# The opening of a recurrent attention stage on Trainium2, written in another order

## What is computed

```python
# r, k, v: (4, 8, 768, 48); w, u: (8, 48)
for t in range(S):
    kt, vt, rt = (k[:, :, t], v[:, :, t], r[:, :, t])
    cur = np.einsum('bhd,bhe->bhde', u[None] * kt, vt)
    y[:, :, t] = np.einsum('bhd,bhde->bhe', rt, state + cur)
    state = w[None, :, :, None] * state + np.einsum('bhd,bhe->bhde', kt, vt)
# y as x: (3072, 384), a row for each token
h = x @ w_in                                   # (3072, 2048)
g = np.where(h >= 1, h, np.where(h <= -1, 0.0, (h + 1) ** 2 / 4))
x = g @ w_out                                  # (3072, 384)
# then a second layer of 8 experts with 1024 columns, one for each token
```

## Time and profile before

| | us |
|---|---|
| median of 3 runs | 768.75 (768.74 to 770.08) |
| the profiled execution | 767.32 |
| its span, first to last instruction | 765.2 |
| TensorE busy | 722.6 (94%) |
| VectorE busy | 407.1 (53%) |
| ScalarE busy | 311.4 (41%) |
| GpSimd busy | 118.6 (16%) |

### The profile page before, as it was taken

How to read it: one execution, slowest core, us unless ns; L and a number is a source line. 1 busy time by engine, 2 the same in 40 slices (tenths; PEclk the granted TensorE clock), 3 DMA queues, 4 the chain that set the end, 5 groups by cost and what they waited for, 6 DMA issues and landing times. The chain is left out here.

```text
span 765.2 us, 12834 instructions
## 1 busy us (share of the span) xinstructions
PE 722.6 (94%) x4947; PEld 607.1 (79%) x4948; DVE 407.1 (53%) x687; ACT 311.4 (41%) x545; POOL 118.6 (16%) x149
## 2 busy tenths in 40 slices
PE   5899999999999999999999999997199999999995
PEld 4688888888888888888888888885089999998995
DVE  6878786755566556655566554543644222223321
ACT  3577665434454445444454446444232212112120
POOL 6300012222221122222222100000520000000000
PEclk9999999999999999999999999999589999999998
DMA  8883122011121111011010001001520120202011
GB/s 151 210 221 74 29 53 64 12 30 33 32 73 32 33 32 56 19 32 32 11 43 2 1 1 42 1 0 43 194 97 21 63 83 1 83 1 82 20 62 41
DMA packets 88317, 40.36 MB, mean 53 GB/s; under 512 B 77113, under 2 KB 84929, under 8 KB 88257
## 3 DMA queue, kind: packets, MB, share of 16 engines
q1 hardware_dynamic: 86400, 34.61, 17.9%
q10 hardware_dynamic: 1856, 4.93, 1.7%
HBM read 30.10 MB, written 9.44 MB: 52 GB/s over the span
## 5 line engine op out<-in xcount | busy, mean ns | idle before, releaser
L946 PE MATMUL x_ps<-g_p,wout_hi 128*128 128x512 f32 x576 | 182.5, 398 | 0.2 <-DVE g_p L726 0.2
L964 PE MATMUL h_ps<-x0T,win_hi 128*128 128x512 f32 x576 | 178.3, 391 | 1.9 <-DVE x0T L654 1.9
L509 ACT ACTIVATE above<-h_ps,minus_one 128x512 f32<-128x512 f32 x96 | 66.0, 688 | 170.0 <-DVE mid L739 169.5
L964 PEld LDWEIGHTS h_ps<-x0T,win_hi 128*128 128x128 f32 x576 | 107.5, 188 | 24.7 <-DVE x0T L654 2.2
L946 PEld LDWEIGHTS x_ps<-g_p,wout_hi 128*128 128x128 f32 x576 | 104.6, 188 | 22.2 <-issue 1.4
L1503 PE MATMUL ch_ps<-x_p,w_p 128*128 128x512 f32 x432 | 109.1, 400 | 12.1 <-DVE w_p L1569 12.1
L739 DVE TENSOR_SCALAR mid<-h_ps 128x512 f32<-128x512 f32 x96 | 66.2, 690 | 98.6 <-PE h_ps L964 98.1
L946 PE MATMUL x_ps<-g_p,wout_lo 128*128 128x512 f32 x288 | 112.6, 391 | 0.0
L964 PE MATMUL h_ps<-x0T,win_lo 128*128 128x512 f32 x288 | 112.1, 389 | 0.0
L748 DVE TENSOR_TENSOR mid<-mid,above 128x512 f32<-128x512 f32 x96 | 70.8, 738 | 70.8 <-ACT mid L510 70.7
L1492 PE MATMUL cy_ps<-w_p,h_p 128*128 128x384 f32 x576 | 107.7, 336 | 0.0
(11 more groups left out here) (214 smaller groups left out, 621.4 us busy)
## 6 DMA issues: line engine op xcount, KB each, us to landing
xr<-xT_scratch SPq DMA_DIRECT2D x8, 768.0 KB, 5.0
rkv<-in_v SPq DMA_DIRECT2D x24, 192.0 KB, 2.9
xT_scratch<-xbuf ACTq DMA_DIRECT2D x6, 768.0 KB, 3.4
out<-acc SPq DMA_DIRECT2D x12, 384.0 KB, 2.4
rkv<-in_r SPq DMA_DIRECT2D x20, 192.0 KB, 3.5
rkv<-in_k SPq DMA_DIRECT2D x20, 192.0 KB, 3.7
win_raw<-in_moe_w_in SPq DMA_DIRECT2D x48, 64.0 KB, 3.3
wout_raw<-in_moe_w_out SPq DMA_DIRECT2D x4, 768.0 KB, 6.8
```

The costliest lines, as they stand in the source:

```text
L509: raises(act.activation(above[:, f % 2], h_ps[f % 2][:, :], ACT.Relu, bias=minus_one[:, :]), "over")
L946: last = pe.matmul(x_ps[kk][:, :], (wout_hi, wout_lo)[a][:, f, cols], g_p[:, at % NG, b], start=(f == 0 and n == 0), stop=(f == NF1 - 1 an ...
L964: last = pe.matmul(h_ps[f % 2][:, :], (win_hi, win_lo)[a][:, f // QF, kk, cols], x0T[:, c % 2, b, kk], start=(kk == 0 and n == 0), stop=(k ...
```

## The change

The block of `make_consts` goes; GpSimd fills `ones` and `ident` inside `stage_ab`, behind the memset of `wq`, with a semaphore `consts_done` for TensorE, and a semaphore `padded` for ScalarE's loads of w. ScalarE writes the diagonals of tiles 0, 1 and 2 one behind the other; that of tile 4 moves from ScalarE to GpSimd. TensorE makes all four y before update(0), and update(1) after h(0); tile 0's state goes to the other h bank, so that update(0) waits for rows_low(0) and h(1), not h(0), for its state. VectorE takes the causal steps and the low parts of y ahead of the scalings of k and the states. GpSimd starts tile 4 after the first win_low.

```diff
@@ make_consts
-    with nc.semaphore("const_filled") as filled, nc.Block() as block:
-        @block.gpsimd
-        def _(pool):
-            pool.memset(ones[:, :], 1.0).then_inc(filled, 1)
-            pool.wait_ge(filled, 1)
-            pool.affine_select(out=ident[:, :], in_=ones[:, :], compare_op=ALU.is_equal, fill=0.0,
-                               base=0, pattern=[[-1, P]], channel_multiplier=1).then_inc(filled, 1)
-            pool.wait_ge(filled, 2)
@@ state_bank, DIAG_ACT
-            return tile_set(it).banks[0] if it < B else l_ps
+            return h_ps[1] if it == 0 else first[it].banks[0] if it < B else l_ps
-        DIAG_ACT = (0, 1, 2, 4, 5, 6, 7)
+        DIAG_ACT = (0, 1, 2, 5, 6, 7)
@@ GpSimd
-                pool.memset(wq[:, 0], 1.0).then_inc(filled, 1)
+                pool.memset(wq[:, 0], 1.0).then_inc(padded, 1)
+                pool.memset(ones[:, :], 1.0).then_inc(consts_done, 1)
+                pool.wait_ge(consts_done, 1)
+                pool.affine_select(out=ident[:, :], in_=ones[:, :], compare_op=ALU.is_equal, fill=0.0,
+                                   base=0, pattern=[[-1, P]], channel_multiplier=1).then_inc(consts_done, 1)
...
                 rest_of_v(3, first_vz[3])
+                pool.wait_ge(win_halved, 1)
                 for it in range(B, NTILE):
@@ ScalarE
-                act.wait_ge(filled, 1)
+                act.wait_ge(padded, 1)
...
                 own_diagonal(1)
+                own_diagonal(2)
                 rows_y(0)
-                own_diagonal(2)
+                split_win(0)
                 rows_y(1)
                 rows_y(2)
-                split_win(0)
                 rows_y(3)
...
-                        if c == 0 and f % 4 == 0:
-                            own_diagonal(it, range(H // 2 if f else 0, H))
+                        if c == 0 and f % 4 == 0 and f:
+                            own_diagonal(it, range(H // 2, H))
@@ VectorE
                 causal(1)
+                own_sum(3)
+                scaled_turned(3)
+                causal(2)
+                rows_low(0)
+                causal(3)
                 dve.wait_ge(tab_k_done, 1)
                 scale_k_late(0)
-                scaled_turned(3)
-                rows_low(0)
-                own_sum(3)
-                causal(2)
+                win_low(0)
+                rows_low(1)
+                rows_low(2)
+                rows_low(3)
                 scale_k_late(1)
-                rows_low(1)
                 next_state(0)
-                causal(3)
-                win_low(0)
-                rows_low(2)
                 scale_k_late(2)
                 scale_k_late(3)
-                rows_low(3)
-                next_state(1)
                 scale_r(B)
-                scale_k(B)
...
                         if c == 0 and f == 0:
+                            own_sum(B)
+                            scale_k(B)
+                            next_state(1)
                             next_state(2)
                             next_state(3)
...
-                        if c == 0 and f == 0:
-                            own_sum(B)
@@ TensorE
                     if it < B:
                         wait(pe, "masked", it)
                         wait(pe, "k_scaled", it)
+                        wait(pe, "x_lo", 0)
...
-                pe.wait_ge(filled, 9)
+                pe.wait_ge(filled, 8)
+                pe.wait_ge(consts_done, 2)
...
                 make_y(1)
+                make_y(2)
+                make_y(3)
                 update(0)
-                make_y(2)
-                update(1)
-                make_y(3)
...
-                        if c == 0 and f == 0:
+                        if c == 0 and f == 1:
                             wait(pe, "stated", 0)
...
                         if c == 0 and f == 0:
+                            update(1)
                             update(2)
                             update(3)
```

More of the change, by code:

```diff
@@ L212, in stage_ab @@
         filled, tabled, biased, blocked = sem("tables_filled"), sem("tables_step"), sem("biases_filled"), sem("blocks_filled")
+        padded, consts_done = sem("w_padded"), sem("consts_done")
         wcol_loaded, u_loaded = sem("wcol_loaded"), sem("u_loaded")
@@ L266, in diagonal_here @@
             elif it >= 0:
-                wait(eng, "diag_done", 0 if it < B else it - 7)
+                wait(eng, "diag_done", (3, 4).index(it) if it <= B else it - 6)
         def own_products(eng, it, to):
@@ L366, in _ @@
                     pool.memset(first_vz[i], 0.0).then_inc(filled, 1)
-                pool.wait_ge(filled, 14)
+                pool.wait_ge(filled, 13)
                 pool.affine_select(out=mask[:, :, :], in_=mask[:, :, :], compare_op=ALU.is_gt, fill=0.0,
@@ L639, in next_state @@
                         wait(dve, "u_done", it)
-                        raises(dve.tensor_tensor(state[:, b], a.banks[0][:, 0:HD], step, ALU.mult), "stated")
+                        raises(dve.tensor_tensor(state[:, b], state_bank(it)[:, 0:HD], step, ALU.mult), "stated")
                         return
@@ L697, in _ @@
                 own_sum(1)
-                dve.wait_ge(filled, 15)
+                dve.wait_ge(filled, 14)
                 causal(0)
@@ L904, in flip_table @@
                     pe.wait_ge(tab_r_done, 1)
-                    pe.wait_ge(filled, 10)
+                    pe.wait_ge(filled, 9)
                     pe.matmul(l_ps[:, 0:HD], flip, flat(tab_r[:, :, :]), start=True, stop=True).then_inc(flipped, 1)
-                pe.wait_ge(filled, 9)
+                pe.wait_ge(filled, 8)
+                pe.wait_ge(consts_done, 2)
                 turn_rk(0)
```

## The result

| | median us | runs | ratio to the kernel before, 95% |
|---|---|---|---|
| kernel before | 768.81 | 4 | |
| changed kernel | 764.37 (763.52 to 764.87) | 4 | 0.9937 (0.9921 to 0.9953) |
| kernel before, later comparison | 768.89 (766.41 to 770.97) | 23 | |
| changed kernel, later comparison | 763.16 (762.44 to 764.54) | 6 | 0.9932 (0.9917 to 0.9948) |

By the medians the change makes the kernel 4.4 us faster in the first comparison and 5.7 in the second; by the ratios it is 4.8 and 5.2. I had forecast 3.2 (765.6), with a range down to 764.4: the direction was right, and the gain was larger than the range allowed for. The two profiled executions differ by less than that: 767.32 and 764.87, 2.45 us. The first is 1.4 us faster than its kernel's median, and the second is the slowest of the ten executions of the changed kernel.

A forecast was written before the change was run, and what follows sets the result against it. Bound: when TensorE's unbroken run begins, at y(4). It moves from 42.78 to 40.65, 2.13 us, plus 1.04 for the earlier start: 3.17 off the median 768.75 gives 765.6 us, range 764.4 to 767.4.

The forecast's parts named there:

- The start: Opening: without the block of constants, first load issued at 0.8, 1.04 us earlier, and what follows moves with it.
- C: Opening: the block's time was hidden behind first-load latency, so no earlier start; gain 2.13, 766.6 us; chance 0.08.
- h(0) at 26.2: TensorE's first matmul of the first layer: 27.2 less 1.04, where it now starts at 30.79.
- h(1) at 31.8: TensorE behind h(0), three updates and transposes: 32.8 on the old clock, 35.52 before.
- The load of w_out as the new bound: ScalarE ahead of h(0)'s functions: split_wout(0) waits for a load landing at 31.1; its 0.93 us stall was covered before.
- The collision: GpSimd's diagonal of tile 4 holds up VectorE's g low; sum of g(1) starts at 38.5, not 37.7: 0.8 us.
- the other two courses: GpSimd's diagonal of tile 4 against VectorE: by the skill's lock rule, a loss of nothing or all of 1.9 us.
- y(4): forecast 39.6: TensorE's y of tile 4, the yardstick: 40.65 on the old clock, 42.78 before; a wait of 0.5 to 1.3 us ahead.
- What lies around the span: Outside the profiled span: 2.1 us between span 765.2 and time 767.32, claimed untouched by the change.
- the gain is a difference inside the program, so I subtract it from the median: Whole kernel: 3.17 us taken from the median 768.75, though the profiled execution was 1.4 faster, giving 765.6.
- rival A: GpSimd's diagonal of tile 4 falls in a hole, no collision: y(4) at 39.85, gain 3.97, 764.8 us; chance 0.2.
- D: ScalarE's new wait for w_out: gain gone if it lands 11 us after issue, 771.3 us at 13.5; chance 0.04.

The follow-up runs named there:

- The run with the diagonal first: Changed kernel with GpSimd's diagonal of tile 4 ahead of the copies of v(4): 763.38 us, ratio 0.9923.
- consts only: Kernel before without the block in make_consts, ones and ident filled inside the stage, order unchanged: 766.84 us, ratio 0.9974.

## Why the prediction was right or wrong

**The start: right.** First issue at 0.79 (forecast 0.8), 1.04 us earlier, and the whole opening with it. C falls.

**h(0) at 26.2: right to 0.5 us.** It started at 26.73, and at 26.27 in the second profile. The half microsecond is the landing of the first quarter of w_in. The split behind it starts at 23.45 in the first profile, with VectorE waiting for it, and at 22.98 in the second; the forecast was 22.96 (24.0 less 1.04).

```profile
23.45 0.84 ACT L425 ACTIVATE win_hi<-win_raw 128x768 fp32r<-128x768 f32 x1 [2.53 <-DMA win_raw<-in_moe_w_in]
24.32 0.96 DVE L671 TENSOR_TENSOR win_lo<-win_raw,win_hi 128x768 fp32r<-128x768 f32 x1 [0.45 <-ACT win_hi L425]
...
22.98 0.84 ACT L425 ACTIVATE win_hi<-win_raw 128x768 fp32r<-128x768 f32 x1 [2.31 <-DMA win_raw<-in_moe_w_in]
```

TensorE's transposes of tile 2, four in 1.06 us and not in 0.6 to 0.74, made causal(0) wait 0.52 for the scores; but they are as slow in the second profile, and the wait for w_in covers them.

**h(1) at 31.8: 1.2 late in the first profile,** 32.98. 0.5 is inherited. The rest comes from three scalings of k and one state on VectorE: beside GpSimd the first scaling takes 1.24 us and the other two 1.38, where I had counted 0.46 for each "with a little more". In the second profile the first scaling takes 0.55, and h(1) starts at 31.91.

**The load of w_out as the new bound: right, and one item short.** The load landed at 30.9 in the first profile and at 29.7 in the second, where I had 30.1; that is most of the 1.09 us between their y(4). The item is missing in "ScalarE would take it, but split_wout(0) is ahead": three issues of loads stand between that split and the function, and they cost 0.59. In the kernel before they were issued while ScalarE was idle, and I read them as free.

**The collision: right in kind, too large in price.** g low(0) took 1.78 and 1.98 us in the two profiles of the changed kernel, the "rest of the diagonal" of the forecast, neither of the other two courses. It ended the wait for the sum of g(1) at 38.39, where ScalarE's square was done at 38.09: 0.3 us and not 0.8, since ScalarE was late as well. The run with the diagonal first shows the same from the other side.

**y(4): forecast 39.6, found at 40.58 and 39.49.** The sum up to here was good to 1 us, and in the first pair of profiles it overstated the gain (2.20 against 3.17).

**What lies around the span: wrong.** "2.1 lie around it and are untouched": it is 1.75 without the block, 0.34 us of gain more. Rows 2 gave no sign of it, as they lie inside the span.

**The step that failed: "the gain is a difference inside the program, so I subtract it from the median".** The profiled execution was 1.4 us below the median, and I took this for noise that has no place. It has one: the profile was of an execution at a mean clock of 0.981, with h(0) at the upper clock, and only 17 of the 71 others are at 0.981. The other 54 have a lower mean clock, and the one of them with a profile loses 1.5 us in h(0), behind its wait of 1.9 us; the changed kernel, with a wait of about 1 us, doesn't. That all 54 lose it in h(0) isn't shown, as only this one has a profile; filling the gap and opening it wider moved the share as it should. Against the median the sum is 2.13 + 1.04 + 0.34 + 1.4 = 4.9, and the runs gave 4.4 and 5.7. The range missed by the same step, as it was built from causes that one profile could show. That the time lies close to rival A's 764.8 speaks for nothing in A: the collision that A leaves out is in both profiles of the changed kernel.

**D, slower:** the load of w_out landed 8.0 us after its issue in the first profile and 7.1 in the second, far from the 11 at which the gain would be gone.

## What to carry to other kernels

When a profiled execution stands apart from the median, look in each run's granted clock for the reason before adding a difference to the median; a wait of TensorE may cost its length and then more, by the clock behind it, in some executions only. A wait on an engine's queue covers more than the next instruction: when it moves, count the issues of loads behind it too. And a barrier at the start can be paid in full by what waits for the first loads, and outside the span as well.

## What the runs showed of the hardware

Behind waits of 1.78 to 2.34 us (TensorE busy for 3.7 to 4.4 of the 7 us from 24 to 31), the granted clock was at its lower level in h(0) in two of the four profiles with such a wait (consts only, the third of the kernel before) and at the upper in the other two; behind 3.88 us it was at the lower one before the wait was over (0.84 in the mean of 26 to 30 us, which TensorE spent waiting), and behind 0.6 to 1.3 us never, in eight profiles. Filling the gap with eight matmuls of no use made the kernel faster by 1.2 us. I had not expected a wait this short to matter. A block with its barrier cost 0.34 us outside the span besides 1.04 in it. Two two-operand instructions in SBUF, on VectorE and GpSimd, that started within 0.1 us of each other took 0.96 and 1.80 us in one execution and 1.75 and 1.00 in another; in both it was the one that started second, by 0.02 and 0.07 us, that took longer.
